# Keys and MLP outputs turned by VectorE in 32x32 blocks and put in place through DRAM, and the first steps in another order

## The reference, cut to what matters

```python
def _attn_ref(r, k, v, w, u):            # each [4, 8, 768, 48]
    for t in range(S):
        cur = einsum('bhd,bhe->bhde', u * k[t], v[t])
        y[t] = einsum('bhd,bhde->bhe', r[t], state + cur)
        state = w[t][..., None] * state + einsum('bhd,bhe->bhde', k[t], v[t])
def _moe_ref(x, w_in, w_out):            # x [3072, 384], w_in [384, 2048]
    h = x @ w_in
    return (h / (1 + exp(-1.702 * h))) @ w_out
def _moe2_ref(x, phi, w1, w2):           # phi [384, 32], w1 [8, 384, 1024]
    logits = x @ phi
    d = softmax(logits over tokens);  slot_input = d.T @ x
    slot_out[e] = max(slot_input[e] @ w1[e], 0) @ w2[e]
    return softmax(logits over slots) @ slot_out
```

## Time and profile before

| | |
|---|---|
| median of 3 runs | 580.77 us |
| profiled execution | 579.11 us, span 577.2 us |
| granted TensorE clock, mean | 0.988 |
| PE (TensorE) busy | 556.0 us, 96% |
| DVE (VectorE) busy | 316.6 us, 55% |
| ACT (ScalarE) busy | 301.1 us, 52% |
| DMA | 80.80 MB in 53733 packets |

### The profile page before, as it was taken

The page is one execution under the profiler, slowest core; times in us unless marked ns, Lnnn a source line. Parts: engine busy times, 40 slices in busy tenths (PEclk is TensorE's granted clock), DMA queues, the critical chain, the costliest instruction groups (busy, mean ns, idle before and its releaser), DMA issues.

```text
span 577.2 us, 15153 instructions
## 1 busy us (share of the span) xinstructions
PE 556.0 (96%) x6279; PEld 508.8 (88%) x6279; DVE 316.6 (55%) x632; ACT 301.1 (52%) x650; POOL 10.3 (2%) x28
## 2 busy tenths in 40 slices
PE   8999889999999999999999999999999999999983
PEld 6889889989989998999999999999999999998332
DVE  8869677757846664566445654664453224323304
ACT  3866636655664445444645474456444456563313
POOL 4010000000000000000000000000000000000000
PEclk9799999999999999999999999999999999999997
DMA  8985623433523331333223422332211396667728
GB/s 284 373 228 182 182 78 108 129 92 103 147 69 98 99 102 49 81 93 108 58 67 97 105 71 76 103 92 70 75 43 30 131 387 227 227 212 266 254 76 327
DMA packets 53733, 80.80 MB, mean 140 GB/s; under 512 B 4304, under 2 KB 33616, under 8 KB 53664
## 3 DMA queue, kind: packets, MB, share of 16 engines
q1 hardware_dynamic: 42160, 54.54, 29.4%
q10 hardware_dynamic: 10704, 22.13, 13.6%
q0 software_dynamic: 800, 3.15, 1.6%
HBM read 70.76 MB, written 9.04 MB: 138 GB/s over the span
## 4 chain that ended last, share of the span: by engine, by line
PE 86%; DVE 5%; DMA 4%; issue 2%; ACT 2%; SPq 0%; DVEq 0%; ACTq 0%
PE hps L1441 33%; PE acc L1576 32%; PE zps L1348 2%; PE mps L1475 2%; PE acc L1690 1%; PE mps L1644 1%; DMA raw<-dmaj 1%; PE mps L1370 1%; PE mps L1657 1%; DMA out<-obuf 1%; PE mps L1677 1%; PE yps L1364 1%; PE mps L1721 1%; PE hps L1721 1%; PE zps L1354 1%
## 5 line engine op out<-in xcount | busy, mean ns | idle before, releaser
L1207 DVE TENSOR_TENSOR gl<-g,gh 128x384 fp32r<-128x384 f32 (+1 forms) x144 | 73.7, 512 | 200.5 <-ACT gh L899 200.0
L1441 PE MATMUL hps<-xh,wi_hi 128*128 128x384 f32 (+1 forms) x432 | 146.2, 338 | 0.7 <-ACT g L888 0.5
L1441 PE MATMUL hps<-xh,wi_lo 128*128 128x384 f32 (+1 forms) x432 | 137.1, 317 | 0.0
L1441 PE MATMUL hps<-xl,wi_hi 128*128 128x384 f32 (+1 forms) x432 | 137.0, 317 | 0.0
L1576 PE MATMUL acc<-wo_hi,gh 128*128 128x384 f32 x384 | 129.3, 337 | 2.3 <-DVE wo_lo L1182 1.6
L1576 PE MATMUL acc<-wo_hi,gl 128*128 128x384 f32 x384 | 129.6, 337 | 0.0
L1576 PE MATMUL acc<-wo_lo,gh 128*128 128x384 f32 x384 | 129.4, 337 | 0.0
L899 ACT ACTIVATE gh<-g 128x384 fp32r<-128x384 f32 (+1 forms) x144 | 70.5, 490 | 106.8 <-PE acc L1576 106.0
L888 ACT ACTIVATE g<-hps 128x384 f32<-128x384 f32 (+1 forms) x144 | 65.6, 456 | 76.2 <-PE hps L1441 74.6
L1441 PEld LDWEIGHTS hps<-xh,wi_hi 128*128 128x128 f32 x432 | 81.1, 188 | 9.2 <-issue 5.3
L1441 PEld LDWEIGHTS hps<-xl,wi_hi 128*128 128x128 f32 x432 | 81.4, 188 | 0.0
(11 more groups left out here) (253 smaller groups left out, 789.2 us busy)
## 6 DMA issues: line engine op xcount, KB each, us to landing
w1s<-w SPq DMA_DIRECT2D x16, 768.0 KB, 6.4
w2s<-w SPq DMA_DIRECT2D x16, 768.0 KB, 6.4
natural<-rknat ACTq DMA_DIRECT2D x21, 384.0 KB, 3.1
vn<-vnat SPq DMA_DIRECT2D x24, 192.0 KB, 2.6
tests<-wall SPq DMA_DIRECT2D x6, 768.0 KB, 12.6
out<-obuf SPq DMA_DIRECT2D x12, 384.0 KB, 3.9
raw<-dmaj ACTq DMA_DIRECT2D x20, 226.2 KB, 2.7
raw<-dmaj ACTq DMA_DIRECT2D x20, 225.8 KB, 2.7
```

The lines of the kernel that those rows point to most:

```text
L1207: dve.tensor_tensor(out=gl[F % 2][:, 0:wide], in0=g32[F % 2][:, 0:wide], in1=gh[F % 2][:, 0:wide].bitcast(fp32), op=ALU.subtract).then_inc ...
L1441: last = pe.matmul(hps[F % 2][:, 0:wide], w[:, g, at:at + 128], v[i % 2][:, g, 0:wide], start=m == 0, stop=m == 3 * G - 1)
```

## The change

From chunk 10 on (`FLIP`) TensorE and ScalarE no longer turn the keys. VectorE transposes kd in 32x32 blocks within itself (`turn_blocks`), SyncE writes the blocks to DRAM in four DMAs, waits for them, and reads them back in four DMAs (runs of 32 floats) as kb, with tokens on partitions and each head pair's 112 rows padded to 128 (`spread_keys`). Sum tiles then have 64 columns of weights in place of 48. For the outputs of steps 2 to 6 (14 chunks) VectorE likewise turns x2 (`turn_x_blocks`), SyncE writes in four DMAs and reads in one (`spread_x`), and the logits read x2b. Slots of `scan`, `invert`, `grow` and loads move by one or two. The rest is the order in the first steps: longer `keep_warm` at three places and none or a shorter one at four, `high_first(1)` ahead of `distances(3)`, `rest_x(0, 0)` ahead of `bound_decays(1)`, and some slots of chunks 2 to 6, of `low_part(7)` and of the first split of x.

```diff
+LONG_WARM = (512,) * 5
+        kb = [sb(f"kb{i}", [C, HP, FB, BLOCK]) for i in range(2)]
+        turned = sb("turned", [128, TB, HP, BLOCK], at=place[0])
+        FLIP = BASE[4] + 1
+        firsts = [BASE[i + 1] + 1 for i in range(3, NST - 1)]
+        BLOCKED = range(2, NST - 2)
-        place_parts(2, scan=1, invert=1, grow=2, weigh=3, decayed=3, turn=4, mask=7, across=6)
+        place_parts(2, scan=1, invert=2, grow=2, weigh=3, decayed=3, turn=4, mask=7, across=6)
-        place_parts(4, load_w=7, load_k=9, load_r=10, load_n=11, scan=13, invert=14, grow=15, weigh=14, decayed=15, turn=16, across=19)
+        place_parts(4, load_w=7, load_k=9, load_r=10, load_n=11, scan=13, invert=14, grow=14, weigh=16, decayed=15, turn=16, across=19)
-        place_parts(6, load_w=19, load_k=20, load_r=21, load_n=22, scan=21, invert=22, grow=22, weigh=25, decayed=24, turn=24, across=27)
+        place_parts(6, load_w=19, load_k=20, load_r=21, load_n=22, scan=21, invert=23, grow=23, weigh=25, decayed=24, turn=25, across=27)
             place_parts(n, load_w=f - 8, load_k=f - 7, load_r=f - 6, load_n=f - 5, scan=f - 6, invert=f - 5, grow=f - 5,
-                        weigh=f - 2, decayed=f - 1, turn=f, across=f + 4)
-            place_parts(n + 1, load_w=f - 2, load_k=f - 1, load_r=f, load_n=f + 1, scan=f + 1, invert=f + 2, grow=f + 3,
-                        weigh=f + 4, decayed=f + 5, turn=f + 5, across=f + 8)
+                        weigh=f - 2, decayed=f, across=f + 4)
+            place_parts(n + 1, load_n=f + 1, weigh=f + 4, decayed=f + 5, across=f + 8)
...
+            else:
+                place_parts(n, flip=f - 4)
+                place_parts(n + 1, load_w=f - 3, load_k=f - 2, load_r=f - 1, scan=f, invert=f + 1, grow=f + 1, flip=f + 1)
+                if not last:
+                    place_parts(n + 2, flip=f + 6)
+            for m, f in zip(range(SIZES[i]), (2, 4, 8)):
+                turn_x_at[NF * (i + 1) + f] = (i, m)
+                spread_x_ahead[BASE[i + 2] + m] = (i, m)
-        low_at = {0: 2, 4: 3, 8: 5, 10: 6, 12: 7}
+        low_at = {0: 2, 4: 3, 8: 5, 10: 6, 11: 7}
-            m = splits[SIZES[i + 1]].get(f) if i else {12: 0, 14: 1}.get(f)
+            m = splits[SIZES[i + 1]].get(f) if i else {13: 0, 14: 1}.get(f)
+            def spread_keys(n):
+                sp.wait_ge(blocks_turned, n - FLIP + 1)
+                for i in range(FB):
+                    sp.dma_start(key_blocks[n % 2, :, :, i].rearrange("j t q -> t j q"),
+                                 turned[BLOCK * i:BLOCK * (i + 1)].rearrange("t j p d -> t j (p d)")).then_inc(blocks_out, 16)
+                sp.wait_ge(blocks_out, 16 * FB * (n - FLIP + 1))
+                sp.wait_ge(meetings, met_in[n - 2])
+                tokens = key_blocks[n % 2].rearrange("j t i (p d) -> p (j t) i d", p=HP)
+                for p in range(HP):
+                    sp.dma_start(kb[n % 2][:, p], tokens[p]).then_inc(kb_in[n % 2], 16)
+            def spread_x(i, m):
+                sp.wait_ge(x_blocks_turned, blocked(i, m))
+                for j in range(TB):
+                    sp.dma_start(x_blocks[m, :, :, j].rearrange("i d q -> d i q"),
+                                 turned_x[BLOCK * j:BLOCK * (j + 1)].rearrange("d i g t -> d i (g t)")).then_inc(x_blocks_out, 16)
+                sp.wait_ge(x_blocks_out, 16 * TB * blocked(i, m))
+                sp.wait_ge(logit_done, i)
+                sp.dma_start(x2b[:, m].rearrange("d j g t -> d (j g t)"),
+                             x_blocks[m].rearrange("i d j q -> (i d) (j q)")).then_inc(x2b_in, 16)
             for n in range(NCH):
...
+                if n + 1 in firsts:
+                    spread_keys(n + 1)
+                keys_ahead = FLIP <= n + 2 < NCH and n + 2 not in firsts
+                if n + 1 in firsts and keys_ahead:
+                    spread_keys(n + 2)
+                if n in spread_x_ahead:
+                    spread_x(*spread_x_ahead[n])
+                if n + 1 not in firsts and keys_ahead:
+                    spread_keys(n + 2)
                 sp.wait_ge(y_done, n + 1)
                 distances(2)
                 excesses(2)
                 high_first(0)
+                high_first(1)
                 distances(3)
-                high_first(1)
                 excesses(3)
+            def turn_blocks(n):
+                dve.wait_ge(front, n + 1)
+                dve.wait_ge(blocks_out, 16 * FB * (n - FLIP))
+                dve.transpose(turned[:, :, :, :].rearrange("t j p d -> t (j p d)"),
+                              kd[n % 2].rearrange("d p (j t) -> d j p t", t=BLOCK)).then_inc(blocks_turned, 1)
                 bound_decays(0)
+                rest_x(dve, 0, 0)
                 bound_decays(1)
-                rest_x(dve, 0, 0)
                 rest_x(dve, 0, 1)
-                                     kn[n % 2][rows, p, HALF * par:HALF * par + D], vn[n % 2][rows, h * D:(h + 1) * D],
+                        keys, features = kb[n % 2][rows, p, 2 * par:2 * par + 2, :].rearrange("t i d -> t (i d)"), HALF
                 state_sums(0)
-                keep_warm(WARM)
+                keep_warm(LONG_WARM)
                 outputs(0)
-                keep_warm(WARM)
+                keep_warm(LONG_WARM)
...
                 state_sums(1)
-                keep_warm(WARM)
+                keep_warm(LONG_WARM)
                 outputs(1)
                 permute(0, permuted)
-                keep_warm(WARM)
                 permute(1, permuted)
-                keep_warm(WARM + WARM)
                 sum_bounds(0)
-                keep_warm(WARM + WARM)
+                keep_warm(WARM)
                 sum_bounds(1)
-                keep_warm(WARM)
+                            pe.wait_ge(kb_in[n % 2], 16 * HP * ((n - FLIP) // 2 + 1))
+                        if i in BLOCKED:
+                            pe.wait_ge(x2b_in, 16 * blocked(i, SIZES[i] - 1))
```

More of the change, by code:

```diff
@@ L23 @@
 HALF = 64
+BLOCK = 32
+FB = 128 // BLOCK
+TB = C // BLOCK
 R = HALF + D
@@ L106, in attention_mlp_soft_experts @@
         rp = [sb(f"rp{i}", [R, HP, C]) for i in range(2)]
-        kd = [sb(f"kd{i}", [R, HP, C]) for i in range(2)]
-        kn = [sb(f"kn{i}", [C, HP, R]) for i in range(2)]
+        kd = [sb(f"kd{i}", [128, HP, C]) for i in range(2)]
+        kn_at = [place[0] + i * FB * HP * BLOCK * 4 for i in range(2)]
+        kn = [sb(f"kn{i}", [C, HP, R], at=kn_at[i]) for i in range(2)]
+        kb = [sb(f"kb{i}", [C, HP, FB, BLOCK]) for i in range(2)]
         natural = sb("natural", [C, 2, DM])
@@ L144, in attention_mlp_soft_experts @@
         x2 = sb("x2", [128, 3, DM])
+        x2t_at = place[0]
         x2t = sb("x2t", [128, G, ST])
+        x2b = sb("x2b", [128, 3, TB, G, BLOCK], at=x2t_at)
         eT = sb("eT", [NG, C])
@@ L262, in attention_mlp_soft_experts @@
         kn_done = sem("kn_done")
+        blocks_turned = sem("blocks_turned")
+        blocks_out = sem("blocks_out")
+        x_blocks_turned = sem("x_blocks_turned")
+        x_blocks_out = sem("x_blocks_out")
+        x2b_in = sem("x2b_in")
+        kb_in = [sem(f"kb_in{i}") for i in range(2)]
         z_done = sem("z_done")
@@ new lines, in attention_mlp_soft_experts @@
+            if not last:
+                place_parts(n + 2, load_w=f + 2, load_k=f + 4, load_r=f + 5, load_n=f + 6, scan=f + 6 - (n >= FLIP),
+                            invert=f + 7 - (n >= FLIP), grow=f + 7 - (n >= FLIP), weigh=f + 8, decayed=f + 9, across=f + 12)
+            if n < FLIP:
+                place_parts(n, turn=f)
+                place_parts(n + 1, load_w=f - 2, load_k=f - 1, load_r=f, scan=f + 1, invert=f + 2, grow=f + 3, turn=f + 5)
+                place_parts(n + 2, turn=f + 9)
+            else:
+                place_parts(n, flip=f - 4)
+                place_parts(n + 1, load_w=f - 3, load_k=f - 2, load_r=f - 1, scan=f, invert=f + 1, grow=f + 1, flip=f + 1)
+                if not last:
+                    place_parts(n + 2, flip=f + 6)
```

81 lines of the change are left out of this document (52 added, 29 removed).

## The result

The changed kernel took 585.32 us (median of 20 runs, 577.84 to 591.03) against 581.0 us of the kernel before in the same job (20 runs, 579.12 to 582.35): a ratio of 1.0048, 95% interval 1.0028 to 1.0068. The forecast was 566. So 2.5% of gain was forecast, and a loss of 0.5% to 0.7% came: the ratio and its interval go by the 14 of the 20 runs that lie within 1.5% of the fastest (their median is 584.18), all 20 give 1.0074, and the profiled execution, 587.80 us with a span of 586.1 us, is one of the other six.

The account below looks back on a forecast made before the run. TensorE, busy throughout a full step, was taken as the bound. 10.2 us from turns plus 4.8 from the start-up less 0.4 for tiles gave 14.6 us gain: 566 us on the median's scale, range 561 to 573.

Parts of the forecast that it names:

- The turns off TensorE: TensorE's middle steps: removing 14 x2 turns saves 4.6 us and 14 kd turns 5.6 us, together 10.2 us.
- Wider sum tiles: TensorE's meetings: weights of 64 instead of 48 columns cost 0 to 2.7 us, taken as 0.4.
- Block transposes on VectorE: VectorE's turns of keys and x2 take 0.7 and 0.55 us each, fitting its free time: cost 0.
- SyncE's queue and the round trip: Steps' DMA queue: spreads ahead of y make its f + 3 store about 5 us late; cost 0 to 1 us in each of 5 steps.
- room and cover: Slack for late y at f + 3: 4.3 us before ScalarE needs x, some 4.5 us in ScalarE's and VectorE's order.
- The fourth rival: SyncE's queue holds y beyond its slack and stops TensorE in each of 5 steps: slower, 587 us; chance 0.05.
- upper end: Reads of kb: at 64 ns per 128-byte run a chunk's keys take 8.2 us, plus 2.7 landing; 2 us was taken.
- The third rival: Keys or x come late and hold the meetings in part: 571 us, or 576 with 2 us waits each; chance 0.12.
- The start-up: First steps: earlier MLP start and shorter waits on VectorE's orders gain 4.8 us, from 2 to 7.
- Both cases: Start-up clock from 20 to 25 us: if held at 2.4 GHz, the first MLP matmul comes at 28.4 us, otherwise 30.3.
- The wait for wo_lo: TensorE's start-up wait in slot 14's output part: an earlier split of x removes it, gaining 1.6 us.
- the first rival: Turns come off as said, but weight DMAs leave the start-up no gain on balance: 571.0 us, 569 to 572; chance 0.15.

Follow-up runs that it names:

- pool_apart: Changed kernel with DRAM spreads issued by GpSimd, x2 turned in slots 2, 8 and 10, third chunk's keys ahead of the second x2: 570.65 us, ratio 0.983.
- x_only: Changed kernel with x2 alone through DRAM, the keys turned by TensorE as before: 572.75 us, ratio 0.9893.
- keys_only: Changed kernel with the keys alone through DRAM, x2 turned by TensorE as before: 575.41 us, ratio 0.9921.
- start_only: Kernel before with only the start-up's edits, no keys or x2 through DRAM: 578.52 us, ratio 0.9972.
- sp_apart: Changed kernel, spreads still on SyncE's queue ahead of y, x2 turned in slots 2, 8 and 10, keys ahead of x2: 609.99 us, ratio 1.0556.

## Why the prediction was wrong, point by point

**The turns off TensorE: right.** All 28 turns lie in slots 48 to 128. In pool_apart these are 7.2 us shorter, although its wide sum tiles cost 1.3 there and the logits 2.0 (7.3 against 5.3 before; it waits for x2b): 10.5 us off TensorE, against 10.2 forecast. By halves it is 4.9 in x_only, against 4.6, and in keys_only 2.8 with 1.3 of wide tiles in them, 4.1 against 5.6.

**Wider sum tiles: under-sized.** 1.3 us in the meetings, forecast 0.4, inside its 0 to 2.7.

**Block transposes on VectorE: right.** All 28 are there, as the groups show, at 0.71 and 0.57 us against 0.7 and 0.55:

```profile
L1138 DVE STREAM_TRANSPOSE turned<-kd 128x512 f32<-128x512 f32 x14 | 9.9, 709 | 0.3
L1145 DVE STREAM_TRANSPOSE turned_x<-x 128x384 f32<-128x384 f32 x14 | 8.0, 573 | 16.9 <-DMA x_blocks<-turned_x 16.9
```

The durations did not hurt. Their waits did, and the prediction had none of them.

**SyncE's queue and the round trip: the step that failed.** It had y at f + 3 about 5 us late and a cost of 0 to 1 us a step. From the end of the key transpose (238.33) to the store of y it took 13.0 us, not 9.7, and the transpose ended 3.9 us ahead of y, not 4.5: so y went out 9.2 us late. By the prediction's own room and cover (4.3 and 4.5 us) that alone would have cost 0.4 us a step, 2 us in all. Four things in it were off. The kb issues took 0.63 us instead of 0.42, and the x_blocks issues up to 1.3, so 12 of them 7.2 us rather than 5.1. The landings of the last stores were 3.2 and 3.0 us instead of 2.1. The third is a wait that it left out: the transpose of x2 at 251.06, held 5.1 us by its own buffer's store. The fourth, which decides, is that it treated the lateness of y, x, keys and v as four sums from a fixed start, where each feeds the next: y at f + 7 was forecast some 3 us late and came 7.8 late (ready at 260.0, stored at 267.78), because VectorE's key turn had itself waited for x. "The load of v has over 10 us of room" was true of a queue in which y's lateness does not add up; 8.6 of TensorE's lost us are waits for v. The fourth rival had the place and the direction (SyncE holds y, 587), and 0.05 for it was far too little; its price, landings of 5 us, was not what did it, and that its 587 lies near the measured 585.3 is luck. Its sum does not come out either: 13 issues at 0.8 us and two landings of 5 are 20.4 us, less 4.5 that makes y 15.9 us late, not 12.

The Trainium skill ("DMA: Bandwidth & Descriptors", Specifications) says that runs under 512 bytes cost a read-modify-write. Here the loads of kb in runs of 128 bytes landed in 3.1 us (the loads of x, 192 KB, in 2.6), well under the forecast's upper end of 8.2 + 2.7. The third rival's mechanism, late keys by slow packets, did not come.

**The start-up: 3.0 instead of 4.8, and a stand not foreseen.** In the profiled execution the clock held at 1.00 from 20 to 25 us and `hidden_layer(0)` began at 28.82; the forecast was 28.4 with the clock up and 30.3 with it down. Both cases came: in 10 of the 15 profiled executions with the new start-up the clock fell at 19 to 21 us for 3.4 us, and `hidden_layer(0)` began at 30.4 to 31.4. So the longer `keep_warm` does not hold the clock reliably. start_only is one of the ten; its window:

```profile
20.00:25.00 5.00, 5.00 (x80) 4.08 (x79) 3.37 (x6) 3.62 (x4) 0.00 (x0) 0.71 1.02 387
```

In the changed kernel the first gelu began at 32.17 behind wi_hi, whose DMA landed at 30.8: 1.8 us ahead of before, as forecast. The wait for wo_lo is gone, that for kd nearly. But TensorE then waits 1.7 to 3.1 us ahead of `hidden_layer(2)`, where it waited 0.5 us before, and in three of the executions stands for 7 us, in which the clock falls to 1.2 GHz, in the changed kernel for 6.8 us. start_only's median is 2.2 us below the kernel before's, about half way between the forecast and the first rival, which had nothing from the start-up.

**The sum.** Forecast -14.6. For the turns and tiles it had -9.8; slots 48 to 128, where they lie, came out 3.5 to 7.7 us longer than before, through the queue's loop. In the profiled execution that was 8.6 us of waits for v, 2.6 for gl and the slower clock behind them. The start-up gave some 2 where it was tried alone; in the profiled execution, with the stand, slot 24 came 1.8 us later than before.

## What to carry to other kernels

A round trip through DRAM that is put on a queue in strict order costs its waits, not its bytes: write down what stands behind each wait, and whether the awaited engine itself waits for something further back in that queue. If it does, lateness feeds itself, and the sum of durations tells nothing. Put such a chain on a queue of its own and keep its single buffers out of the fast engine's way; here the same work then went from 585.3 to 570.7 us.

## What the runs showed of the hardware

- Four DMAs into kb, each of 512 runs of 128 bytes, took 0.63 us apiece to issue on SyncE's queue (a store of y took 0.44 there) and 0.75 on GpSimd's (2.98 for four).
- In mid-kernel the clock fell to 1.2 GHz behind or within waits of TensorE of 1.87 and 3.07 us, for 3.4 and 6.8 us. A wait of 2.07 us at 209.7, in the same execution, had no fall behind it.
- The same DMAs in the same order took 330.8 us for five steps when SyncE issued them ahead of y, v and x, and 294.8 when GpSimd did (sp_apart and pool_apart).
- TensorE stood 7 us ahead of a branch, with the packet of instructions at 35.6 to 36.6 us, in 3 of the 15 profiled executions with the new start-up. What decides stays open.
